# Layer 1's down step with seven block products for some pairs, and ELU from Relu and Exp

## Chip, cores and metric

The kernel runs on one core of a Trainium2 chip. The metric is the time of one execution in microseconds (us) of device time, and lower is better. The kernel before takes 1011.63 us, the median of three runs (1011.47 to 1011.79).

## The reference

There are 6016 tokens and 256 channels. An attention over channels comes first: q and k are divided by their column norms, `a = softmax(k^T q / tau)` is 256x256, and the tokens become `v @ a`. Two layers follow, each with 2048 hidden columns:

```python
h = x @ w_in                                   # [6016,256] @ [256,2048]
g = where(h > 0, h, exp(minimum(h, 0)) - 1)    # layer 1: ELU;  layer 2: g = h / (1 + exp(-h))
y = g @ w_out                                  # [6016,2048] @ [2048,256]
```

All is float32. TensorE (PE) works on `fp32r` operands. Each operand is split in two parts, hi (rounded) and lo (the rest), and a product is three matmuls: hi hi, hi lo and lo hi (`PARTS`).

## The kernel before

`a` is folded into layer 1's first weights (`a_w_in1 = a @ w_in1`, eight pieces), so that layer 1 starts at v itself. Layer 1 runs over 12 token tiles, ten of 512 tokens and the last two of 448 (`ONE`). Its hidden columns are 16 f blocks of 128. One tile and one f block make a unit.

For each unit, PE runs `up` (2 channel blocks times 3 parts, six matmuls of 512 columns, into one of four PSUM banks). ScalarE (ACT) writes Exp of the bank to `g_raw` (L728). VectorE (DVE) takes `min(e, 1) - 1` (L953) and then `max(h, 0) + that` (L957). ACT copies the result, rounded, to the hi part (`g_hi`, L700), and DVE subtracts for the lo part (`g_lo`, L911). Three units later PE runs `down`: for two output blocks c, three matmuls each, summed over all 16 f blocks in the tile's own bank (six matmuls of 512 columns). So a unit is 12 matmuls, and PE's order is up(f), down(f-3), up(f+1), down(f-2). ACT and DVE have loops of their own over the same units and do other work in fixed slots: the split of the finished tile's output (`y1_hi_of`, `y1_lo_of`), the transposition and split of the next tile of v (`v_transpose`, `vT_hi`, `vT_lo`), in tile 0 the split of seven more weight pieces (`weights_hi`, `weights_lo`, slots `SLOTS_WEIGHTS`), in tiles 1 to 4 two pairs each of the weight sums that layer 2 needs (`form_sums`, `form_hi`, `form_lo`). Every engine takes its instructions in order; semaphores join them.

Layer 2 (`TWO`, six double tiles) takes f blocks in pairs and already computes its down step with seven products of half-size blocks in place of eight (a Strassen-Winograd scheme): sums of g quarters (`pair_sums`) and of weight blocks (`w_out2_forms`) are multiplied, and sums of the seven results (`c_sums`) give the outputs. Its pairs go through a ring of four weight buffers that SyncE (SP) loads.

Of the kernel before, what the change touches and what calls it, by code (L numbers as in the profile page):

```python
# [63 lines left out]
M7, M5, M6, M4, M1, M2, M3 = range(N_PRODUCTS)  # L64

# [8 lines left out]
FIRST_H = (0, 1, 2, 3, 4, 0, 4, 5)  # L74
# [7 lines left out]
def build(nc, q, k, v, tau, w_in1, w_out1, w_in2, w_out2, out):  # L82
# [16 lines left out]
    assert N % P == 0 and C == 2 * P and F % WC == 0 and FB % N_H == 0  # L99

    ctx = ExitStack()
    with ctx:
# [16 lines left out]
        xb = [[place(f"x_parts{b}{a}", [P, 2, CB, T], F32R) for a in range(2)] for b in range(2)]  # L119
# [34 lines left out]
        assert at_wout1 + 2 * N_PRODUCTS * T * 4 <= at_x and at_g + 2 * N_PRODUCTS * T * 4 <= at_y1
        cursor[0] = at_x
        ring += [place(f"w_forms{r}", [P, N_PRODUCTS, 2, P], F32R) for r in range(1, N_RING)]
        assert cursor[0] <= at_g
        cursor[0] = at_g + 2 * N_PRODUCTS * T * 4
        mc = place("m_tile", [P, N_PRODUCTS + 2, T], F32)
        o_sb = place("out_tile", [P, 2, G, CB, BLK], F32)  # L160
# [4 lines left out]
        wraw = place("early_w_in1_parts", [P, 2, CB, F], F32R, at_win2_parts)  # L165

# [3 lines left out]
        cursor[0] = at_g  # L170
# [93 lines left out]
        class Phase:  # L264
# [21 lines left out]
        for t in range(NT):  # L286
            ONE.append(Phase(t // 2, t % 2, T_LAST if t >= NT - 2 else T, ONE[-1] if ONE else None))
# [3 lines left out]
        IN_LOOP_1, IN_LOOP_2 = range(6, NT - 4), range(1, NU - 1)  # L291
        assert len(IN_LOOP_1) % 2 == len(IN_LOOP_2) % 2 == 0

        def phases_one(eng, one):

            for ph in ONE[:IN_LOOP_1[0]]:
                one(ph)
            with eng.Fori(0, len(IN_LOOP_1) // 2) as i:
                half = i + IN_LOOP_1[0] // 2
                a = Phase(half, 0, before=Phase(half - 1, 1))  # L300
                one(a)
                one(Phase(half, 1, before=a))
            for ph in ONE[IN_LOOP_1[-1] + 1:]:
                one(ph)
# [22 lines left out]
        unit = lambda ph, f: ph.tile * FB + f  # L327

# [120 lines left out]
        def _(sp):  # L449
# [96 lines left out]
            weight_load(IN2 + 2)  # L546
            weight_load(IN2 + 3)
            v_load(2)
            form_load(0)
            for t in range(1, IN_LOOP_1[0]):  # L550
                spill(t - 1)
                if 2 * t - 1 < PAIRS:
                    form_load(2 * t - 1)
                    form_spill(2 * t - 2)
                v_load(t + 2)
                if 2 * t <= PAIRS:
                    if 2 * t < PAIRS:
# [69 lines left out]
        def _(act):  # L627
# [70 lines left out]
            def g_hi(ph, f):  # L698
                act.wait_ge(u_g, unit(ph, f) + 1)
                act.activation(gp[:, f % N_H, 0, 0:ph.n], g_sb[:, f % 2, 0:ph.n], ACT.Copy).then_inc(u_hi, 1)  # L700

            def y1_hi_of(ph):


                if ph.fixed == 0:
                    act.wait_ge(w_split, n_split(IN2 + N_PIECES - 1))
                else:
                    act.wait_ge(d_spill, 16 * ph.tile)
                for c in range(CB):
# [12 lines left out]
            def phase_one(ph):  # L722
                for f in range(FB):
                    act.wait_ge(u_up, unit(ph, f) + 1)

                    if not (ph.fixed == 0 and f < 2):
                        act.wait_ge(u_lo, unit(ph, f) - 1)
                    act.activation(g_sb[:, f % 2, 0:ph.n], h_ps[f % N_H][:, 0:ph.n], ACT.Exp).then_inc(u_act, 1)  # L728
                    if shifted(ph, f, 1):
                        g_hi(*shifted(ph, f, 1))  # L730
                    if f == SLOT_EVICT and ph.before:
                        y1_hi_of(ph.before)
                    if f == SLOT_V + 1 and ph.v_next:
                        vT_hi(*ph.v_next)
                    if weights_in_slot(ph, f) is not None:
                        weights_hi(act, weights_in_slot(ph, f))
                    if f and pair_in_slot(ph, f - 1) is not None:
                        form_hi(pair_in_slot(ph, f - 1))

            phases_one(act, phase_one)  # L740
# [36 lines left out]
            def tile(u):  # L777
                for k in range(PAIRS):
                    back = shifted(u, k, 1, PAIRS)
                    if u is TWO[0] and k == 0:  # L780
                        g_hi(ONE[-1], FB - 1)
# [10 lines left out]
                    if u is TWO[0] and k == 1:  # L792
                        y1_hi_of(ONE[-1])
# [524 lines left out]
```

## Time and profile before

| | us |
|---|---|
| median of three runs | 1011.63 |
| profiled execution | 1011.59 |
| its span, first to last instruction | 1009.8 |
| PE busy | 1004.0 (99%) |
| PE weight loads (PEld) busy | 894.7 (89%) |
| DVE busy | 781.7 (77%) |
| ACT busy | 577.2 (57%) |

Busy time is the union of an engine's instructions. A matmul's record is longer than the step to the next matmul, since matmuls overlap in the array. DVE and ACT instructions overlap a little too, so the step from start to start is shorter than the duration.

### The profile page before, as it was taken

The page shows a single profiled execution, that of the slowest core. Times are in us where ns is not written, and L with a number is a line of the kernel's source. Part 1 is how long each engine was busy: PE and PEld are TensorE (multiplying, and loading weights), DVE is VectorE, ACT ScalarE, POOL GpSimd, SP SyncE. Part 2 cuts the span into 40 slices and gives each one's busy share as a digit, 9 for nine tenths or more (in the row PEclk, how much of TensorE's full clock was granted, in tenths as well). Part 3 has the DMA queues.
Part 4 walks back from the last instruction along what each step waited for, and adds up shares of the span by engine and source line. Part 5 has one row for each costly group of instructions (what it writes and reads, how often), then busy time and mean ns, then how long its engine had stood idle before and what let it go on. Part 6 is the DMA issues. An engine that isn't in the chain of part 4 may idle for free.

```text
span 1009.8 us, 13274 instructions
## 1 busy us (share of the span) xinstructions
PE 1004.0 (99%) x4750; PEld 894.7 (89%) x4750; DVE 781.7 (77%) x1106; ACT 577.2 (57%) x916; POOL 10.2 (1%) x11
## 2 busy tenths in 40 slices
PE   9999999999999999999999999999999999999998
PEld 8888888888888888889999888888888888888997
DVE  7789878778777776777775866877887886886886
ACT  6766555555544444454445656656666665666664
POOL 0300000000000000000000000000000000000000
PEclk9999999999999999999999999999999999999999
DMA  9912313233111121114103325236237236334333
GB/s 350 373 17 73 110 53 104 102 102 110 74 27 43 21 63 42 19 53 175 42 37 146 110 74 192 89 92 238 73 95 229 93 93 203 109 93 130 110 97 91
DMA packets 115062, 109.77 MB, mean 109 GB/s; under 512 B 89024, under 2 KB 97216, under 8 KB 112448
## 3 DMA queue, kind: packets, MB, share of 16 engines
q1 hardware_dynamic: 114400, 108.58, 33.2%
q8 instruction: 32, 0.52, 0.2%
q10 hardware_dynamic: 608, 0.49, 0.2%
q14 instruction: 22, 0.18, 0.1%
HBM read 83.23 MB, written 25.82 MB: 108 GB/s over the span
## 4 chain that ended last, share of the span: by engine, by line
PE 97%; DMA 1%; ACT 1%; DVE 0%; issue 0%; SPq 0%; DVEq 0%
PE bank L1110 73%; PE bank L1257 21%; PE bank L1120 2%; DMA early_w_in<-w_in 1%; DMA early_qk<-k 0%; PE bank L1289 0%; ACT g_pair L751 0%; ACT g_pair_parts L758 0%; PE bank L1297 0%; DVE m_tile L1089 0%; ACT g_pair_parts L765 0%; SPq L461 0%; ACT early_w_in_parts L368 0%; PE bank L1153 0%; DVE out_tile L1100 0%
## 5 line engine op out<-in xcount | busy, mean ns | idle before, releaser
L1110 PE MATMUL bank<-g_parts,w_out_parts 128*128 128x512 f32 (+1 forms) x1152 | 274.9, 375 | 0.0
L1110 PE MATMUL bank<-x_parts,w_in_parts 128*128 128x512 f32 (+1 forms) x1152 | 274.5, 375 | 0.2 <-ACT g_pair L751 0.2
L1110 PE MATMUL bank<-xT_parts,a_w_in 128*128 128x512 f32 (+1 forms) x1152 | 274.5, 375 | 0.0
L728 ACT ACTIVATE g_raw<-bank 128x512 f32<-128x512 f32 (+1 forms) x192 | 112.8, 588 | 234.5 <-PE bank L1110 222.8
L1110 PEld LDWEIGHTS bank<-x_parts,w_in_parts 128*128 128x128 f32 x1152 | 215.9, 189 | 28.5 <-ACT g_pair L751 1.0
L1110 PEld LDWEIGHTS bank<-xT_parts,a_w_in 128*128 128x128 f32 x1152 | 217.9, 189 | 25.8
L1110 PEld LDWEIGHTS bank<-g_parts,w_out_parts 128*128 128x128 f32 x1152 | 218.0, 189 | 25.5
L1257 PE MATMUL bank<-g_pair_parts,w_forms 128*128 128x512 f32 (+1 forms) x987 | 239.3, 375 | 0.0
L1257 PEld LDWEIGHTS bank<-g_pair_parts,w_forms 128*128 128x128 f32 x987 | 186.8, 189 | 21.9
L751 ACT ACTIVATE g_pair<-bank 128x512 f32<-128x512 f32 (+1 forms) x192 | 112.9, 588 | 133.8 <-PE bank L1110 126.6
L953 DVE TENSOR_SCALAR g_raw<-g_raw 128x512 f32<-128x512 f32 (+1 forms) x192 | 80.2, 418 | 93.1 <-ACT g_raw L728 92.2
L911 DVE TENSOR_TENSOR g_parts<-g_raw,g_parts 128x512 fp32r<-128x512 f32 (+1 forms) x192 | 130.4, 679 | 12.8 <-ACT g_parts L700 0.8
L997 DVE TENSOR_TENSOR g_pair_parts<-g_forms,g_pair_parts 128x1024 fp32r<-128x1024 f32 (+1 forms) x96 | 115.1, 1200 | 21.6 <-ACT g_pair_parts L758 21.6
L957 DVE SCALAR_TENSOR_TENSOR g_raw<-bank,g_raw 128x512 f32<-128x512 f32 (+1 forms) x192 | 129.2, 673 | 0.0
L758 ACT ACTIVATE g_pair_parts<-g_forms 128x1024 fp32r<-128x1024 f32 (+1 forms) x96 | 99.2, 1035 | 34.4 <-PE bank L1257 33.3
L700 ACT ACTIVATE g_parts<-g_raw 128x512 fp32r<-128x512 f32 (+1 forms) x192 | 117.8, 614 | 1.2 <-DVE g_raw L957 1.2
L984 DVE TENSOR_TENSOR g_forms<-g_pair 128x1024 f32<-128x1024 f32 (+1 forms) x48 | 57.7, 1202 | 66.3 <-ACT g_pair L751 66.2
L1003 DVE TENSOR_TENSOR g_pair_parts<-g_pair,g_pair_parts 128x1536 fp32r<-128x1536 f32 (+1 forms) x48 | 82.5, 1718 | 2.0 <-ACT g_pair_parts L765 2.0
L765 ACT ACTIVATE g_pair_parts<-g_pair 128x1024 fp32r<-128x1024 f32 (+1 forms) x96 | 78.8, 822 | 0.6 <-PE bank L1257 0.6
L1120 PE MATMUL bank<-early_qk 128*128 128x256 f32 x188 | 41.3, 380 | 0.2 <-DMA early_qk<-k 0.2
L1120 PEld LDWEIGHTS bank<-early_qk 128*128 128x128 f32 x188 | 35.6, 191 | 5.1 <-DMA early_qk<-q 0.4
L821 DVE TENSOR_TENSOR early_square_sums<-early_square_sums,early_squares 128x1024 f32<-128x1024 f32 (+1 forms) x24 | 28.9, 1203 | 8.3 <-ACT early_squares L645 6.1
(84 smaller groups left out, 358.2 us busy)
## 6 DMA issues: line engine op xcount, KB each, us to landing
w_forms<-w_forms SPq DMA_DIRECT2D x48, 896.0 KB, 4.7
y_parts<-y1T_parts SPq DMA_DIRECT2D x10, 1024.0 KB, 3.9
x_parts<-y_parts SPq DMA_DIRECT2D x10, 1024.0 KB, 8.5
w_forms<-w_out_forms SPq DMA_DIRECT2D x8, 896.0 KB, 4.8
early_qk<-q SPq DMA_DIRECT2D x23, 256.0 KB, 7.4
early_qk<-k SPq DMA_DIRECT2D x22, 256.0 KB, 7.8
out<-out_tile SPq DMA_DIRECT2D x40, 128.0 KB, 2.7
v_in<-v SPq DMA_DIRECT2D x36, 128.0 KB, 3.4
```

The source lines that it names most:

```text
L700: act.activation(gp[:, f % N_H, 0, 0:ph.n], g_sb[:, f % 2, 0:ph.n], ACT.Copy).then_inc(u_hi, 1)
L728: act.activation(g_sb[:, f % 2, 0:ph.n], h_ps[f % N_H][:, 0:ph.n], ACT.Exp).then_inc(u_act, 1)
L751: act.activation(g2[:, k % 2, i, 0:u.n], h_bank(u, k, i)[:, 0:u.n], ACT.Silu).then_inc(u_act, 1)
L758: act.activation(gp2[k % 2][:, 0, 3 + 2 * s:5 + 2 * s, 0:u.n], t_sb[:, 2 * s:2 * s + 2, 0:u.n], ACT.Copy).then_inc(t_hi, 1)
L911: dve.tensor_tensor(part(1), g_sb[:, f % 2, 0:ph.n], part(0).bitcast(F32), ALU.subtract).then_inc(u_lo, 1)
L953: dve.tensor_scalar(g, g, 1.0, 1.0, ALU.min, ALU.subtract).then_inc(u_em, 1)
L957: dve.scalar_tensor_tensor(g, h_ps[f % N_H][:, 0:ph.n], 0.0, g, ALU.max, ALU.add).then_inc(u_g, 1)
L997: dve.tensor_tensor(part(1), t_sb[:, 2 * s:2 * s + 2, 0:u.n], part(0).bitcast(F32), ALU.subtract).then_inc(t_lo, 1)
L1003: dve.tensor_tensor(part(1), g2[:, k % 2, 1:4, 0:u.n], part(0).bitcast(F32), ALU.subtract).then_inc(r_lo, 1)
L1110: mm = pe.matmul(dst, lhsT, rhs, start=first and n == 0, stop=last and n == len(todo) - 1)
L1120: mm = pe.matmul(s_ps[i][:, 0:C], qk[c % NQ][:, K, r, i * P:(i + 1) * P], qk[c % NQ][:, Q, r, :], start=c == 0 and r == 0, stop=c == NCH - ...
L1257: mm = pe.matmul(m_banks[m][:, 0:u.n], ring[k % N_RING][:, form, x, :], by_turns(gp2[k % 2][:, y, operand, 0:u.n]), start=k == 0 and part ...
```

## The change

Layer 1 now works in pairs of f blocks, eight slots to a tile, and PE's lag is two pairs. Tile 0 has no pair with seven products; tiles 1 to 8 have three (pairs 0, 2, 4), tiles 9 to 11 four (0, 2, 4, 6). The others are plain: 12 down matmuls of a full tile. A pair with seven products takes the tile's two token halves and the pair's two f blocks as quarters of g (256 columns each, 224 in the last two tiles). DVE makes four sums of quarters (`one_sums`), ACT rounds three quarters and the four sums, DVE makes their lo parts, and PE runs 21 matmuls of 256 columns. The seven results lie in halves of banks 4 to 7; ACT copies one bank (`one_copy`), DVE makes the output halves (`y_sums`) and adds the plain pairs' sums (`y_rows`). The four weight sums for four pairs are made once, in tile 0 (`one_forms_*`).

ELU becomes: ACT writes `relu(-h)` (`relu`), then `exp(-that)` in place (`exp`), and DVE takes `max(e - 1, h)` for the whole pair in one instruction of 1024 elements (`one_g`).

Layer 2's weight sums move from two pairs a tile in tiles 1 to 4 to one a tile in tiles 1 to 8. The loops of layer 1 are written out. Several buffers move, and with them the first loads of layer 2: the tokens of its second tile wait for the last output of layer 1, its first two ring loads for layer 1's last pair but one, the next two for its last pair.

```diff
-SLOTS_WEIGHTS = (1, 3, 5, 8, 10, 12, 14)
+SLOTS_WEIGHTS = (1, 2, 3, 4, 5, 6, 7)
+SLOT_ONE_FORMS_SUM, SLOT_ONE_FORMS_HI, SLOT_ONE_FORMS_LO = 5, 6, 7
-FORM_PHASES = (1, 2, 3, 4)
+FORM_PHASES = (1, 2, 3, 4, 5, 6, 7, 8)
+SLOT_FORM_SUM, SLOT_FORM_HI, SLOT_FORM_LO = 0, 2, 6
+SLOT_V_TURN, SLOT_V_HI, SLOT_V_LO = 4, 5, 6
+SLOT_ROWS, SLOT_Y1_HI, SLOT_Y1_LO = 2, 3, 4
+COPY_LAG, SUM_LAG = 3, 4
+ONE_PRODUCTS = (M1, M5, M7, M6, M2, M3, M4)
+WINO_FEW, WINO_MORE = (0, 2, 4), (0, 2, 4, 6)
-FIRST_H = (0, 1, 2, 3, 4, 0, 4, 5)
+FIRST_H = (0, 1, 2, 3, 0, 1, 2, 3)
...
+            def relu(ph, k, i):
+                f = 2 * k + i
+                act.wait_ge(u_up, unit(ph, f) + 1)
+                if one_pair(ph, k) >= 2:
+                    act.wait_ge(u_lo, 2 * one_pair(ph, k) - 2)
+                act.activation(raw_units(ph, k)[:, i, :], h_ps[f % 4][:, 0:ph.n], ACT.Relu, scale=-1.0).then_inc(u_relu, 1)
+            def exp(ph, k, i):
+                act.wait_ge(u_relu, unit(ph, 2 * k + i) + 1)
+                e = raw_units(ph, k)[:, i, :]
+                act.activation(e, e, ACT.Exp, scale=-1.0).then_inc(u_act, 1)
+            def normal_hi(ph, k):
+                act.wait_ge(u_g, one_pair(ph, k) + 1)
+                pair_free(ph, k)
+                act.activation(gpn[k % 2][:, 0, :, 0:ph.n], raw_units(ph, k), ACT.Copy).then_inc(u_hi, 2)
...
+            def slot_one(ph, k):                       # ScalarE
+                if ph.tile == 1 and k == SLOT_ROWS:
+                    y1_hi_of(ONE[0])
+                back = shifted(ph, k, 1, PAIRS)
+                is_wino = back is not None and back[1] in back[0].wino
+                if is_wino:
+                    one_plain_hi(*back)
+                relu(ph, k, 0)
+                if is_wino:
+                    one_sums_hi(*back)
+                elif back:
+                    normal_hi(*back)
+                exp(ph, k, 0)
+                relu(ph, k, 1)
+                exp(ph, k, 1)
...
+                if ph.tile > 1 and k == SLOT_Y1_HI:
+                    y1_hi_of(ph.before)
+                if k == SLOT_V_HI and ph.v_next:
+                    vT_hi(*ph.v_next)
+                if weights_in_slot(ph, k) is not None:
+                    weights_hi(act, weights_in_slot(ph, k))
+                if ph.tile == 0 and k == SLOT_ONE_FORMS_HI:
+                    one_forms_hi()
...
+            def one_g(ph, k):
+                dve.wait_ge(u_act, unit(ph, 2 * k + 1) + 1)
+                g = raw_units(ph, k)
+                dve.scalar_tensor_tensor(g, g, -1.0, two_banks[k % 2][:, :, 0:ph.n], ALU.add, ALU.max).then_inc(u_g, 1)
...
+            def slot_one(ph, k):                       # VectorE
+                back = shifted(ph, k, 1, PAIRS)
+                if ph.tile == 1 and k == SLOT_ROWS:
+                    y1_lo_of(ONE[0])
+                if back:
+                    one_g(*back)
+                for tile in (ph, ph.before):
+                    if tile and tile.wino and k + PAIRS * (tile is not ph) == tile.wino[-1] + SUM_LAG:
+                        y_sums(tile)
+                if ph.tile > 1 and k == SLOT_ROWS:
+                    y_rows(ph.before)
+                if back:
+                    one_pair_parts(*back)
+                if ph.tile > 1 and k == SLOT_Y1_LO:
+                    y1_lo_of(ph.before)
+                if k == SLOT_V_TURN and ph.v_next:
+                    v_transpose(*ph.v_next[:2])
+                if k == SLOT_V_LO and ph.v_next:
+                    vT_lo(*ph.v_next)
+                if weights_in_slot(ph, k) is not None:
+                    weights_lo(dve, weights_in_slot(ph, k))
+                if ph.tile == 0 and k == SLOT_ONE_FORMS_SUM:
+                    one_forms_sums()
+                if ph.tile == 0 and k == SLOT_ONE_FORMS_LO:
+                    one_forms_lo()
+                if form_pair(ph) is not None and k == SLOT_FORM_SUM:
+                    form_sums(form_pair(ph))
+                if form_pair(ph) is not None and k == SLOT_FORM_LO:
+                    form_lo(form_pair(ph))
...
+                if f % 2 == 0 and one_pair(ph, f // 2) >= 2:        # TensorE, up()
+                    pe.wait_ge(u_g, one_pair(ph, f // 2) - 1)
...
+            for ph in ONE:
+                for k in range(PAIRS):
+                    up(ph, 2 * k)
+                    up(ph, 2 * k + 1)
+                    if shifted(ph, k, LAG_PAIRS, PAIRS):
+                        one_down(*shifted(ph, k, LAG_PAIRS, PAIRS))
```

`one_sums` is three DVE instructions of 512, 256 and 256 elements that wait for each other, `one_plain_lo` two (512, 256), `one_sums_lo` one of 1024; `one_plain_hi` and `one_sums_hi` are their ACT counterparts. `normal_lo` is one DVE instruction of 1024. `y_sums` is 256, 256 and 512 elements, one waiting for the other, `y_rows` twice 512. `one_forms_sums` is four instructions of 512, `one_forms_hi` and `one_forms_lo` two each of 1024.

## Rows read from the trace of the kernel before

**Rows 1.** The page's first part: busy us (share) x instructions of each engine.
```profile
PE 1004.0 (99%) x4750; PEld 894.7 (89%) x4750; DVE 781.7 (77%) x1106; ACT 577.2 (57%) x916; POOL 10.2 (1%) x11
```
**Rows 2.** The page's chain that ended last, by engine.
```profile
PE 97%; DMA 1%; ACT 1%; DVE 0%; issue 0%; SPq 0%; DVEq 0%
```
**Rows 3.** Busy time by stretch: us, PE, PEld, DVE, ACT, POOL, clock, DMA, GB/s.
```profile
58.50:100.00 41.50, 41.50 (x194) 36.40 (x193) 37.92 (x62) 27.01 (x43) 0.00 (x0) 1.00 0.18 45
341.40:382.90 41.50, 41.50 (x194) 36.36 (x194) 30.50 (x53) 19.94 (x37) 0.00 (x0) 1.00 0.14 39
```
**Rows 4.** PE's timeline in layer 1: start, us, what (512 and 448 columns).
```profile
352.45 1.46 PE L1110 MATMUL bank<-xT_parts,a_w_in 128*128 128x512 f32 x6
355.04 1.46 PE L1110 MATMUL bank<-xT_parts,a_w_in 128*128 128x512 f32 x6
...
537.58 1.30 PE L1110 MATMUL bank<-xT_parts,a_w_in 128*128 128x448 f32 x6
539.85 1.30 PE L1110 MATMUL bank<-xT_parts,a_w_in 128*128 128x448 f32 x6
```
**Rows 5.** The timeline of short matmuls and of weight loads in the early stage.
```profile
47.03 1.04 PE L1153 MATMUL bank<-ident,v_in 128*128 128x128 f32 x8
...
40.69 0.63 PEld L1131 LDWEIGHTS bank<-ones,early_square_sums 128*128 128x128 f32 x4
41.24 4.62 PEld L1120 LDWEIGHTS bank<-early_qk 128*128 128x128 f32 x22
```
**Rows 6.** Groups by shape: line engine op, shapes, count, busy us, mean ns.
```profile
L1110 PEld LDWEIGHTS bank<-g_parts,w_out_parts 128*128 128x128 f32 x1152 | 218.0, 189 | 25.5
L1120 PE MATMUL bank<-early_qk 128*128 128x256 f32 x188 | 41.3, 380 | 0.2 <-DMA early_qk<-k 0.2
L1153 PE MATMUL bank<-ident,v_in 128*128 128x128 f32 x8 | 1.0, 272 | 0.0
```
**Rows 7.** ACT's timeline in layer 1, tile 7 and tile 0.
```profile
351.36 0.60 ACT L728 ACTIVATE g_raw<-bank 128x512 f32<-128x512 f32 x1 [1.48 <-PE bank L1110]
351.85 0.62 ACT L700 ACTIVATE g_parts<-g_raw 128x512 fp32r<-128x512 f32 x1
352.37 1.07 ACT L711 ACTIVATE y1T_parts<-bank 128x512 fp32r<-128x512 f32 x2
...
62.34 1.04 ACT L368 ACTIVATE w_out_parts<-early_w_out 128x1024 fp32r<-128x1024 f32 x1
63.28 0.58 ACT L728 ACTIVATE g_raw<-bank 128x512 f32<-128x512 f32 x1
```
**Rows 8.** DVE's timeline in layer 1, tile 7, and in layer 2.
```profile
351.99 0.43 DVE L953 TENSOR_SCALAR g_raw<-g_raw 128x512 f32<-128x512 f32 x1 [0.78 <-ACT g_raw L728]
352.51 0.69 DVE L911 TENSOR_TENSOR g_parts<-g_raw,g_parts 128x512 fp32r<-128x512 f32 x1
353.12 0.68 DVE L957 SCALAR_TENSOR_TENSOR g_raw<-bank,g_raw 128x512 f32<-128x512 f32 x1
...
647.05 1.23 DVE L997 TENSOR_TENSOR g_pair_parts<-g_forms,g_pair_parts 128x1024 fp32r<-128x1024 f32 x1 [0.53 <-ACT g_pair_parts L758]
648.20 1.22 DVE L1026 TENSOR_TENSOR m_tile<-m_tile 128x1024 f32<-128x1024 f32 x1
```
**Rows 9.** Groups by shape on DVE and ACT, shorter ones, and a table load.
```profile
L943 DVE TENSOR_TENSOR w_out_forms<-form_stage,w_out_forms 128x256 fp32r<-128x256 f32 x8 | 3.4, 419 | 0.0
L929 DVE TENSOR_TENSOR w_out_form_sums<-form_stage 128x128 f32<-128x128 f32 x8 | 2.3, 284 | 0.0
L997 DVE TENSOR_TENSOR g_pair_parts<-g_forms,g_pair_parts 128x896 fp32r<-128x896 f32 x16 | 17.3, 1089 | 2.8 <-ACT g_pair_parts L758 2.8
L751 ACT ACT_TABLE_LOAD x1 | 1.3, 1283 | 0.0
```
**Rows 10.** Waits in tile 0 (58 to 101 us): total, times, longest.
```profile
ACT g_raw L728 <- DVE g_parts L911: 11.7, 9, 1.5
```
**Rows 11.** The page's DMA issues: count, KB each, us to landing.
```profile
w_forms<-w_forms SPq DMA_DIRECT2D x48, 896.0 KB, 4.7
```

More of the change, by code:

```diff
@@ L154, in build @@
[L154 to L158, printed above, removed]
+        assert cursor[0] <= at_forms1
+        ring = [place(f"w_forms{r}", [P, N_PRODUCTS, 2, P], F32R) for r in range(2)]
+        assert cursor[0] <= at_e
+        cursor[0] = at_e
+        ring += [place(f"w_forms{r}", [P, N_PRODUCTS, 2, P], F32R) for r in range(2, N_RING)]
@@ L290, in build @@
         LAST = TWO[-1]
[L291 to L304, printed above, removed]
+        IN_LOOP_2 = range(1, NU - 1)
+        assert len(IN_LOOP_2) % 2 == 0
         def tiles_two(eng, one):
@@ L702, in y1_hi_of, with one_copy @@
+            def one_copy(ph):
+                act.wait_ge(p1_down, one_pair(ph, ph.wino[-1]) + 1)
+                if ph.tile >= 2:
+                    act.wait_ge(y1_lo, CB * ph.tile)
+                act.activation(y_sum(ph, slice(Y_P1, Y_P5 + 1, Y_P5 - Y_P1)),
+                               bank[4][:, 0:ph.n].rearrange("p (s x) -> p s x", s=2), ACT.Copy).then_inc(m1_copy, 1)
             def y1_hi_of(ph):
-                if ph.fixed == 0:
+                if ph.tile == 0:
                     act.wait_ge(w_split, n_split(IN2 + N_PIECES - 1))
+                    act.wait_ge(p1_down, PAIRS)
@@ L714, in form_hi, with one_forms_hi @@
+            def one_forms_hi():
+                act.wait_ge(f1_sum, 4)
+                for i in range(2):
+                    act.activation(forms1[:, 2 * i:2 * i + 2, :, 0, :], form1_raw[:, 2 * i:2 * i + 2, :, 1, :],
+                                   ACT.Copy).then_inc(f1_hi, 1)
             def form_hi(k):
@@ L720, in form_hi @@
                 act.activation(forms[:, b, A11, 0, :], form_stage[:, 0, 0, :], ACT.Copy).then_inc(f_hi, 1)
[L722 to L738, printed above, removed]
@@ L973, in pair_sums @@
+            for ph in ONE:
+                for k in range(PAIRS):
+                    slot_one(ph, k)
             def pair_sums(u, k, step):
@@ L1049, in tile @@
                     if u is TWO[0] and k == 0:
-                        g_lo(ONE[-1], FB - 1)
+                        one_g(ONE[-1], PAIRS - 1)
+                        one_pair_parts(ONE[-1], PAIRS - 1)
+                    if u is TWO[0] and k == 1:
+                        y_sums(ONE[-1])
                     if back:
@@ L1071, in tile @@
                         plain_lo(*back)
-                    if first:
+                    if u is TWO[0] and k == 3:
                         y1_lo_of(ONE[-1])
```

397 lines of the change are left out of this document (268 added, 129 removed).

## The prediction, made before the changed kernel was run

> **What bounds the kernel now.** I read the page's engine shares first, then the chain that ended last, then busy time by stretch. PE is busy for 1004.0 of 1009.8 us [rows 1], and 97% of the chain is PE [rows 2]: the reader is to see that a change pays only through PE's matmuls, and costs only what makes PE wait. In layer 1 PE is busy in every microsecond of a tile [rows 3], at the full 2.4 GHz clock. Twelve matmuls of 512 columns take 355.04 - 352.45 = 2.59 us, 0.216 each; twelve of 448 take 2.27 us, 0.189 each [rows 4]. So a tile of 16 units is 41.4 us, one of the last two 36.3. In those 41.4 us DVE has 30.5 us of work and ACT 19.9; in tile 0 DVE has 37.9 [rows 3], and ACT waits nine times for DVE's lo parts there [rows 10]. The two are not idle helpers: I take them as the second bound.
>
> **PE's part.** A pair with seven products replaces 12 matmuls of 512 columns by 21 of 256. No row has an fp32r matmul of 256 columns, so I bound its step. From below: eight short PE transpositions, of 272 ns each [rows 6], step by (1.04 - 0.27) / 7 = 0.110 us [rows 5], each with its own weight load; the straight line through the 512 and 448 column steps (0.027 us per 64 columns) gives 0.109 at 256. From the weight loads: the four of L1131 belong to matmuls of one column, so nothing but the loads can space them. From the first of them (40.69) to the next group (41.24) are 0.55 us; the first waits out one fp32 matmul (0.216, 41.3 us over 188 is 0.220 [rows 6]), the other three are (0.55 - 0.216) / 3 = 0.111 us apart [rows 5]. From above: a load's own record, 0.189 us [rows 6]. I take 0.111, where the nearest rows meet. Then a pair is 21 x 0.111 = 2.33 instead of 2.59: 0.26 us gained, in 8 x 3 + 4 = 28 pairs 7.2 us. With 224 columns the load's 0.111 stays the floor: 2.33 against 2.27, 0.06 lost in each of 8 pairs. One plain matmul a tile is cut in two, under 0.01 us. PE alone would gain 7.2 - 0.5 = 6.7 us.
>
> One rule of the Trainium skill speaks against even this. "Perfetto Trace Analysis", section "Identifying the Most-Contended Engine", judges TensorE's headroom by the summed time of its LDWEIGHTS records. By it 21 x 0.189 = 3.97 us would be the cost of a pair, and the change a loss. The rows do not bear it out: four records of 0.19 fit in 0.63 us [rows 5], so records overlap and their sum is no occupancy. It is the third rival.
>
> **What ACT and DVE now have to do in a slot.** An instruction occupies its engine from start to start: ACT 0.49 us for 512 elements from a bank, 0.52 from SBUF, 0.94 for 1024; its result is there after 0.60, 0.62, 1.05 [rows 7]. DVE: 0.61 and 1.15, results after 0.69 and 1.22 [rows 8]; 256 elements give 0.42, 128 give 0.28 [rows 9]. A hand-over takes 0.03 (ACT ends at 351.96, DVE starts at 351.99 [rows 7, 8]). ELU by itself costs ACT one pass of 0.52 more a unit and saves DVE 0.34 + 0.61 - 0.575. Both engines have that time; what they don't have is the order. `one_g(k)` waits for `exp(k,1)`; ACT puts `normal_hi(k-1)` or `one_sums_hi(k-1)`, which wait for DVE, ahead of `exp(k,0)`, `relu(k,1)`, `exp(k,1)`. So from one `one_g` to the next there is a closed ring through both engines, and its length is the least time of a slot:
> - plain slot: one_g 1.22 + 0.03, normal_hi 0.94, exp 0.52, relu 0.60 + 0.03, exp 0.62 + 0.03 = 3.99 us;
> - slot with seven products: one_g 1.25, the three sums one after the other (0.69 + 0.42 + 0.42, with 0.03 each) 1.62, one_sums_hi 0.94, then 0.52 + 0.63 + 0.65 as above = 5.61 us.
>
> PE needs 5.18 for a plain slot and 2.59 + 2.33 = 4.92 for the other. The ring is longer in every slot with seven products.
>
> **Tiles 1 to 8.** Slot 0 is DVE's own: one_g 1.15, y_sums 1.51 (0.45 + 0.45 + 0.61), normal_lo 1.15, four form sums at 0.21 = 4.65. Slots 1, 3, 5: 5.61 each, 16.83. Slots 2 and 7: 3.99 each. In slots 4 and 6 DVE's queue is the length, since behind normal_lo (one_g 1.25, normal_hi 1.05 + 0.03, normal_lo 1.15, and 0.15 because y1_hi or vT_hi pushes normal_hi back) stand y1_lo 1.22 and v_transpose 1.15, or vT_lo 1.22 and form_lo 1.16: 6.0 each. The sum is 4.65 + 16.83 + 7.98 + 12.0 = 41.5 us. PE would need 41.43 - 3 x 0.26 = 40.65. So the tile is as long as before, +0.1: the matmuls' gain is spent waiting for `u_lo` and `u_g`. In 8 tiles +0.5 us. With hand-overs of 0.06 instead of 0.03 the eleven later tiles lose some 9 us more; with none they win 9.
>
> **Tile 0.** Here each of slots 1 to 7 has a weight piece, and it joins the ring: behind `exp(k,1)` ACT does weights_hi, DVE's weights_lo waits for that, and `one_g(k)` stands behind it. The ring is 1.25 + 0.94 + 0.52 + 0.63 + 0.52 + 1.05 + 0.03 + 1.15 = 6.09 us, while PE needs 5.18. Slot 5 adds vT_hi (1.04, ahead of weights_hi) and one_forms_sums (0.61 + 0.61 + 0.72 + 0.61 = 2.55): 9.68. Slot 7 adds one_forms_lo (2 x 1.15): 8.39. The seven are 4 x 6.09 + 9.68 + 6.09 + 8.39 = 48.5, for PE 36.3. There is no lead to eat into, because `up` of pair 2 already waits for `one_g(0)` (no down step lies between pairs 0, 1 and 2). So +12.2 us. Cover that is gone: before, PE's `up` didn't wait for `u_g` and the pieces lay seven in sixteen slots. In tile 1 PE's first product in banks 6 and 7 waits for y1_lo of tile 0, which follows its last down by two passes on each engine: +1.0.
>
> **Tiles 9 to 11.** Tile 9: four slots of 5.61, two of 4.0, one of 6.0, one of 4.85 (slot 6 without forms): 41.3, -0.1. Tiles 10 and 11: instructions of 896 instead of 1024 elements save 0.13 [rows 9], those of 448 0.07, so the slots are 5.1 (four), 3.6, 4.5 (y_sums and y_rows together), 5.3 and 4.3: 38.2 against 36.3, twice +1.9 = +3.8.
>
> **Layer 2's start and SP.** The last tile's plain hi, y_sums and y_rows (1.51 + 1.22 and 0.9 us more than before) now lie beside layer 2's first slots. Ring loads 0 and 1 start with the end of layer 1's last seven-product pair, about 7.4 us before layer 2's first down, and take 4.7 [rows 11]; the second double tile's tokens, now behind the last spill, have a whole double tile. I take +1 us, between 0 and +4. On SP `v_load(2)` now stands ahead of the last weight load, but both wait for tile 0's slots 4 and 5 and are used after 7. The form loads, one a tile, wait for nothing late.
>
> Relu has no row. If it shared no table with Exp, each switch would be 1.28 us [rows 9], hundreds of us in all. Copy stands between Exps in every unit without one. The Trainium skill, "ScalarE: Activation LUTs", section "Table sets: the hidden batching unit", has relu in every set; no run here shows it. I take nothing.
>
> **Sum.** 12.2 + 1.0 + 0.5 - 0.1 + 3.8 + 1.0 = +18.4 us. PE's own gain of 6.7 is inside these tile lengths. The profiled execution took 1011.59 (span 1009.8), the median is 1011.63: 1030.0.
>
> **The rivals.**
> - *Only tile 0 pays* (chance 0.15). Later tiles run at PE's pace, because the ring is 2% over it and a little more overlap than I read takes that away. -6.7 + 12.2 + 1.0 + 1.0 = +7.5: 1019. For it: the margin is 0.85 us a tile. Against it: every term is a mean with little spread.
> - *Faster* (0.11): the ring binds nowhere, tile 0's pieces hide as they do now (seven pieces, PE busy throughout [rows 3]), and PE gets its 6.7 less 0 to 1: 1005. It decides at slot 1 of tile 0: if one_g's step there is under 5.18. Against it: that ring is read off the order of instructions.
> - *Short matmuls are dear* (0.10). If loads of 0.189 space them, PE needs 41.43 + 3 x 1.38 = 45.6 in tiles 1 to 8 (+33), +5.5 in tile 9, +1.7 x 8 = 13.6 in the last two, with tile 0 and the rest 1077. Or only 224 columns are dear: run like plain fp32, in four passes (256 columns take two records of 0.216 each, [rows 6]), a step of 0.432 x 224 / 256 = 0.378, 21 of them 7.9 instead of 2.27, +41: 1071.
> - *Table switches* (0.02): over 1100.
>
> The forecast itself has 0.62, from 1019 to 1042 by the hand-overs and layer 2's start. **Range** 1010 to 1042: it takes in the first rival, and leaves out the faster case and the dear ones. No change means within 0.2%, 2 us, about what a measurement of this kernel can tell. Faster by more 0.12, within 0.03, slower by more 0.85.
>
> **What would show it.** Starts of one_g in tile 0 6.1 us apart, and PE idle there for some 12 us, with DVE as releaser; tile length 41.5 in tiles 2 to 8, with PE idle 0.8 us a tile; 21 short matmuls in 2.33 us; no more table loads than three; the last two tiles 38 each. The prediction is wrong if PE is busy throughout tile 0, or if short matmuls step by more than 0.12.

## The result and the profile after

The changed kernel takes 1069.97 us (median of four runs, 1068.86 to 1070.87) against 1011.71 for the kernel before on the same chip: ratio 1.0574 [1.0556, 1.0593], 58.3 us slower. The prediction was 1030.0, slower by 18.4, with a range up to 1042. The direction is right, the size isn't.

The page's first part and its chain, beside [rows 1] and [rows 2]:
```profile
PE 1023.8 (96%) x5085; PEld 904.8 (85%) x5085; DVE 831.3 (78%) x963; ACT 722.0 (68%) x1097; POOL 10.2 (1%) x11
...
PE 42%; DVE 23%; ACT 15%; issue 9%; DVEq 0%; ACTq 0%
```
PE no longer is the bound: the chain's share of PE fell from 97% to 42%, and DVE and ACT carry 38%. Busy time by stretch, with the columns of [rows 3]; the first stretch is tile 0 and tile 1, the second the rest of layer 1 but its last slots, the third layer 2's start:
```profile
58.00:160.00 102.00, 92.82 (x434) 78.14 (x434) 72.35 (x86) 70.46 (x111) 0.00 (x0) 0.97 0.17 46
160.00:580.00 420.00, 394.29 (x2104) 350.48 (x2103) 338.24 (x444) 310.28 (x510) 0.00 (x0) 0.98 0.19 57
580.00:640.00 60.00, 55.26 (x271) 48.39 (x270) 43.74 (x50) 38.47 (x57) 0.00 (x0) 0.97 0.22 85
```
PE idles 9.2, 25.7 and 4.7 us in these stretches. What PE waited for, total, times and longest:
```profile
PE banks L1314 <- DVE g_raw L1015: 23.2, 14, 4.2
PE banks L1452 <- DVE g_form_parts L1049: 5.6, 7, 1.1
PE banks L1452 <- DVE y_sums L1084: 3.9, 9, 0.6
PE banks L1314 <- ACT g_pair L850: 2.6, 3, 1.7
PE banks L1314 <- ACT g_raw L749: 2.1, 1, 2.1
```
In the first line `up` waits for `one_g` (L1015), from which the prediction counts its slots. These are, from start to start of `one_g`:

| tile | slots 0 to 7, us | sum | forecast |
|---|---|---|---|
| 0 | 6.17 6.14 6.14 6.15 9.71 6.15 8.41 4.53 (`one_g` of pairs 0 to 7) | 53.4 | 6.09, 9.68, 8.39 named |
| 3 | 4.73 5.65 4.07 5.65 **9.37** 5.62 6.02 4.05 | 45.2 | 4.65 5.61 3.99 5.61 **6.0** 5.61 6.0 3.99 = 41.5 |

Tiles 2 to 7 are alike within 0.3 us. From `one_g` of pair 0 to that of the next tile, tile 8 takes 44.5, tile 9 44.5, tile 10 41.3. Seven of tile 3's eight slots are within 0.1 us of the forecast. Slot 4 is not: 9.3 to 9.4 for 6.0, in tiles 2 to 9. In tile 10 it takes 7.5, in tile 11 6.0, both for a forecast of 5.3.

PE's timeline around such a slot (tile 5), beside [rows 4] and [rows 5]:
```profile
310.77 0.50 PE L1452 MATMUL banks<-g_form_parts,w_out_parts 128*128 128x256 f32 x3
...
313.11 2.76 PE L1314 MATMUL banks<-xT_parts,a_w_in 128*128 128x512 f32 x12
315.70 2.75 PE L1428 MATMUL banks<-g_parts,w_out_parts 128*128 128x512 f32 x12
320.35 2.86 PE L1314 MATMUL banks<-xT_parts,a_w_in 128*128 128x512 f32 x12 [1.90 <-DVE g_raw L1015]
```
The 21 short matmuls of a pair take 313.11 - 310.77 = 2.34 us, 0.111 each, as forecast. Then PE is idle for 1.90 us until `one_g` at 319.13 has ended. The two engines ahead of it, ACT and DVE, beside [rows 7] and [rows 8]:
```profile
309.60 2.78 ACT L791 ACTIVATE y1T_parts<-y_sums 128x512 fp32r<-128x512 f32 x2
312.29 0.58 ACT L744 ACTIVATE g_raw<-banks 128x512 f32<-128x512 f32 x1
312.77 1.05 ACT L759 ACTIVATE g_parts<-g_raw 128x1024 fp32r<-128x1024 f32 x1
```
```profile
309.73 1.22 DVE L1015 SCALAR_TENSOR_TENSOR g_raw<-g_raw,banks 128x1024 f32<-128x1024 f32 x1 [0.44 <-ACT g_raw L749]
313.92 1.23 DVE L1020 TENSOR_TENSOR g_parts<-g_raw,g_parts 128x1024 fp32r<-128x1024 f32 x1 [2.97 <-ACT g_parts L759]
315.06 2.98 DVE L1090 TENSOR_TENSOR y1T_parts<-y_sums,y1T_parts 128x512 fp32r<-128x512 f32 x2
317.97 1.22 DVE L939 STREAM_TRANSPOSE v_transposed<-v_in 128x1024 f32<-128x1024 f32 x1
319.13 1.17 DVE L1015 SCALAR_TENSOR_TENSOR g_raw<-g_raw,banks 128x1024 f32<-128x1024 f32 x1
```
`y1_hi` (L791) takes 2.78 us for two passes, where [rows 7] has 1.07; it holds back `normal_hi` (L759), so DVE is idle for 2.97. Then `y1_lo` (L1090) takes 2.98 for two. The operation, the number of elements and the step of the read (every fourth element, 16 bytes) are those of before. What differs is where they read: before, a PSUM bank; now `y_sums`, in SBUF. Tile 0 of the changed kernel has no `y_sums`; its output is still read from the banks, with the same step, by the same two lines, which take there what they took before:
```profile
121.89 1.07 ACT L791 ACTIVATE y1T_parts<-banks 128x512 fp32r<-128x512 f32 x2
122.51 1.29 DVE L1090 TENSOR_TENSOR y1T_parts<-banks,y1T_parts 128x512 fp32r<-128x512 f32 x2 [0.92 <-ACT y1T_parts L791]
```

### The profile page after: what moved, and what is told of

Same layout as the page of the kernel before. It is cut to its first block, busy times and chain, and to the rows that moved or that the text cites. A ratio compares the mean times of both kernels' runs of the same rounds, so it can differ in the third digit from the quotient of the medians.

```text
span 1069.1 us, 14152 instructions
## 1 busy us (share of the span) xinstructions
PE 1023.8 (96%) x5085; PEld 904.8 (85%) x5085; DVE 831.3 (78%) x963; ACT 722.0 (68%) x1097; POOL 10.2 (1%) x11
## 4 chain that ended last, share of the span: by engine, by line
PE 42%; DVE 23%; ACT 15%; issue 9%; DVEq 0%; ACTq 0%
PE banks L1314 22%; PE banks L1511 19%; ACT g_raw L749 6%; DVE g_raw L1015 5%; ACT g_raw L744 3%; DVE g_parts L1020 3%; ACT y1T_parts L791 2%; DVE g_raw_forms L1031 2%; ACT g_parts L759 2%; DVE y1T_parts L1090 2%; DVE g_form_parts L1043 2%; DVE g_raw_forms L1034 1%; DVE g_raw_forms L1036 1%; DVE v_transposed L939 1%; DVE g_form_parts L1044 1%
## 5 line engine op out<-in xcount | busy, mean ns | idle before, releaser
L1314 PE MATMUL banks<-xT_parts,a_w_in 128*128 128x512 f32 (+1 forms) x1152 | 271.3, 387 | 23.3 <-DVE g_raw L1015 23.2
L1314 PE MATMUL banks<-x_parts,w_in_parts 128*128 128x512 f32 (+1 forms) x1152 | 276.4, 376 | 4.7 <-ACT g_pair L850 2.6
L1314 PEld LDWEIGHTS banks<-xT_parts,a_w_in 128*128 128x128 f32 x1152 | 220.3, 195 | 56.9 <-DVE g_raw L1015 26.4
L1314 PEld LDWEIGHTS banks<-x_parts,w_in_parts 128*128 128x128 f32 x1152 | 215.9, 190 | 34.6 <-ACT g_pair L850 4.5
L1511 PE MATMUL banks<-g_pair_parts,w_forms 128*128 128x512 f32 (+1 forms) x987 | 239.3, 375 | 0.0
L1511 PEld LDWEIGHTS banks<-g_pair_parts,w_forms 128*128 128x128 f32 x987 | 186.5, 189 | 22.1
L850 ACT ACTIVATE g_pair<-banks 128x512 f32<-128x512 f32 (+1 forms) x192 | 112.9, 588 | 134.6 <-PE banks L1314 127.8
L1428 PE MATMUL banks<-g_parts,w_out_parts 128*128 128x512 f32 (+1 forms) x709 | 162.6, 376 | 0.0
L1428 PEld LDWEIGHTS banks<-g_parts,w_out_parts 128*128 128x128 f32 x709 | 133.7, 190 | 16.3
L1015 DVE SCALAR_TENSOR_TENSOR g_raw<-g_raw,banks 128x1024 f32<-128x1024 f32 (+1 forms) x96 | 114.5, 1193 | 25.0 <-ACT g_raw L749 25.0
L1020 DVE TENSOR_TENSOR g_parts<-g_raw,g_parts 128x1024 fp32r<-128x1024 f32 (+1 forms) x60 | 72.4, 1207 | 69.1 <-ACT g_parts L759 68.6
L749 ACT ACTIVATE g_raw<-g_raw 128x512 f32<-128x512 f32 (+1 forms) x192 | 118.1, 615 | 3.1
L759 ACT ACTIVATE g_parts<-g_raw 128x1024 fp32r<-128x1024 f32 (+1 forms) x60 | 62.6, 1043 | 56.0 <-issue 47.8
```

What stands on the lines that cost most here:

```text
L749: act.activation(e, e, ACT.Exp, scale=-1.0).then_inc(u_act, 1)
L759: act.activation(gpn[k % 2][:, 0, :, 0:ph.n], raw_units(ph, k), ACT.Copy).then_inc(u_hi, 2)
L850: act.activation(g2[:, k % 2, i, 0:u.n], h_bank(u, k, i)[:, 0:u.n], ACT.Silu).then_inc(u_act, 1)
L1015: dve.scalar_tensor_tensor(g, g, -1.0, two_banks[k % 2][:, :, 0:ph.n], ALU.add, ALU.max).then_inc(u_g, 1)
L1020: dve.tensor_tensor(part(1), raw_units(ph, k), part(0).bitcast(F32), ALU.subtract).then_inc(u_lo, 2)
L1314: mm = pe.matmul(dst, lhsT, rhs, start=first and n == 0, stop=last and n == len(todo) - 1)
```

## The experiments

**Is it the way `y_sums` is read?** e1 reads it in order and leaves out the turn of the tokens that the output needs. e2 keeps the turn: it reads `y_sums` in order and writes with a step of 512 bytes; its `y1_lo` also reads the hi part with that step.
```diff
-    act.activation(y1T[...].rearrange("p (m b) -> p m b", m=4), turned_back(y_raw(ph, c), 4), ACT.Copy)
+    # e1, tiles from 1 on; y1_lo alike
+    act.activation(y1T[...].rearrange("p (m b) -> p m b", m=4), y_raw(ph, c).rearrange("p (m b) -> p m b", m=4), ACT.Copy)
+    # e2
+    act.activation(y1T[...].rearrange("p (m b) -> p b m", m=4), y_raw(ph, c).rearrange("p (b m) -> p b m", m=4), ACT.Copy)
```


> The changed kernel, with the two passes that split a layer 1 output tile (y1_hi, y1_lo) reading it in order instead of every fourth element; the tokens' order within tiles 1 to 11 is left out, all else is the same. Theory (the passes themselves are dear, because they now read SBUF with a step of 16 bytes: 1.41 and 1.48 us instead of 0.59 and 0.68 from a bank): the passes fall to about 0.62 and 0.69, slot 4 (one_g to one_g) from 9.4 to 6.0 us, tiles 2 to 8 from 45.2 to 41.6, in all 31 us less: 1039. Rival (slot 4 is long because ACT and DVE stand in the wrong order, and because PE's clock falls): passes shorter, but slot 4 stays above 8 us, and the time above 1060.

> The changed kernel, whole, with the same two passes reading the tile in order and writing y1T with a step of 512 bytes between neighbours (the lo pass also reads the hi part with that step). If only reading with a step of 16 bytes is dear, the passes are 0.62 and 0.69 us and the time is that of the kernel without the turn, 1039. If any step in SBUF costs this much, the time stays at 1070.

Measured: e1 1035.8 us, ratio to before 1.024 [1.0223, 1.0257]; e2 1052.51, 1.0402 [1.0385, 1.042]. The groups of the passes (count, busy us, mean ns), in after, e1 and e2:
```profile
L791 ACT ACTIVATE y1T_parts<-y_sums 128x512 fp32r<-128x512 f32 (+1 forms) x22 | 29.0, 1368 | 0.0
L1090 DVE TENSOR_TENSOR y1T_parts<-y_sums,y1T_parts 128x512 fp32r<-128x512 f32 (+1 forms) x22 | 30.4, 1426 | 0.0
```
```profile
L793 ACT ACTIVATE y1T_parts<-y_sums 128x512 fp32r<-128x512 f32 (+1 forms) x22 | 12.3, 604 | 0.0
L1094 DVE TENSOR_TENSOR y1T_parts<-y_sums,y1T_parts 128x512 fp32r<-128x512 f32 (+1 forms) x22 | 13.9, 673 | 0.0
```
```profile
L796 ACT ACTIVATE y1T_parts<-y_sums 128x512 fp32r<-128x512 f32 (+1 forms) x22 | 21.9, 1098 | 0.0
L1099 DVE TENSOR_TENSOR y1T_parts<-y_sums,y1T_parts 128x512 fp32r<-128x512 f32 (+1 forms) x22 | 22.2, 1053 | 0.0
```
With the turn gone, slot 4 is 6.05 us and tile 3 41.85: 34 us of the 58 are the strided read. e2 lies between both expectations: ACT's pass, whose write alone has a step, takes 1.10 us, so a step on the writing side costs too, though less (slot 4 7.65).

**Is the step dear by itself?** e4 is the kernel before with eight DVE subtractions and eight ACT copies of 512 elements added behind its end, one after the other, reads with steps of 4, 8, 16, 32, 64 and 512 bytes and writes with 16 and 512.
```diff
+    dve.tensor_tensor(t_out(way), g_in(way), t_two(way), ALU.subtract)    # way: the step
+    act.activation(t_out(way), g_in(way), ACT.Copy)
```


> The kernel before, and behind its end on DVE eight subtractions and on ACT eight copies of 512 elements, one after the other: reading with steps of 4, 8, 16, 32, 64 and 512 bytes between neighbours, then writing with steps of 16 and 512. Its total time means nothing. Theory (a step of 16 bytes in SBUF reads is dear): the first two near 0.69 (DVE) and 0.62 (ACT), 16 bytes near 1.45 and 1.4. Open: the steps above 16 bytes, and the writes. Rival (the passes are slow in the changed kernel because other engines use the same memory at the time): all eight near 0.69 and 0.62 here.

Steps of 4, 8 and 16 bytes on DVE, then on ACT:
```profile
1006.59 0.68 DVE L1127 TENSOR_TENSOR g_forms<-g_pair 128x512 f32<-128x512 f32 x1
1007.30 0.69 DVE L1129 TENSOR_TENSOR g_forms<-g_pair 128x512 f32<-128x512 f32 x1
1008.03 1.06 DVE L1131 TENSOR_TENSOR g_forms<-g_pair 128x512 f32<-128x512 f32 x1
```
```profile
1014.52 0.63 ACT L820 ACTIVATE g_forms<-g_pair 128x512 f32<-128x512 f32 x1 [8.47 <-DVE g_forms L1141]
1015.18 0.66 ACT L822 ACTIVATE g_forms<-g_pair 128x512 f32<-128x512 f32 x1
1015.87 1.11 ACT L824 ACTIVATE g_forms<-g_pair 128x512 f32<-128x512 f32 x1
```
Every larger step, read or written, took 1.01 to 1.12 us. So a step of 16 bytes costs 0.38 on DVE and 0.48 on ACT, and a larger one about as much, in one execution with PE idle. That explains e2's passes, and only half (DVE) or some 60% (ACT) of what after's passes take more than e1's. In after itself the passes are shorter where PE's matmuls have 448 columns. Tile 9's lie in tile 10 (below); tile 10's, of 448 elements, lie in tile 11 and take 1.02 and 0.98 us each, while those of tile 11, also of 448 elements, lie in layer 2 beside matmuls of 512 columns and take 1.35 and 1.38.
```profile
534.58 2.19 ACT L791 ACTIVATE y1T_parts<-y_sums 128x512 fp32r<-128x512 f32 x2
539.15 2.11 DVE L1090 TENSOR_TENSOR y1T_parts<-y_sums,y1T_parts 128x512 fp32r<-128x512 f32 x2
```

**Who slows them further?** e8 puts PE beside them: four streams of matmuls behind the end of the kernel before. The kernel's matmuls read their moving operand interleaved, alternately from its first and its second half.
```diff
+    for n, turned, count in ((512, True, 60), (448, True, 68), (512, False, 60), (256, True, 116)):
+        x = gp2[0][:, 0, j % N_PRODUCTS, 0:n]
+        pe.matmul(bank[0][:, 0:n], ring[0][...], by_turns(x) if turned else x, ...)
```


> Edit: the kernel before, whole, and behind its last output four streams of fp32r matmuls on PE: 60 of 512 columns in the interleaved order of the kernel (its two runs 1024 bytes apart), 68 of 448 so (896 bytes apart), 60 of 512 in plain order, 116 of 256 interleaved. Beside each stream ACT makes four copies of 512 elements, then DVE four subtractions: twice with a 16-byte read step, once with a 512-byte step, once in order. Alone (PE idle) these took 1.11, 1.11, 1.08, 0.63 on ACT and 1.06, 1.06, 1.03, 0.68 on DVE; in the changed kernel the 16-byte passes took 1.41 and 1.48 beside matmuls of 512 columns and 1.10 and 1.06 where the last two tiles' matmuls of 448 ran. Theory A (the interleaved stream of 512 columns slows a read of 16-byte step, and the distance of its two runs matters): 1.4 and 1.5 in the first stream, 1.1 in the others. Theory B (any PE stream does it): 1.4 and 1.5 in all four. Theory C (it isn't PE's reads, but the other engine or the DMA queues of the running kernel): 1.1 in all four.

The first read of 16-byte step in each stream, on ACT and on DVE:
```profile
1008.71 1.59 ACT L826 ACTIVATE g_forms<-g_pair 128x512 f32<-128x512 f32 x1 [2.07 <-PE bank L1331]
...
1021.53 1.15 ACT L826 ACTIVATE g_forms<-g_pair 128x512 f32<-128x512 f32 x1 [7.81 <-PE bank L1331]
...
1034.60 1.11 ACT L826 ACTIVATE g_forms<-g_pair 128x512 f32<-128x512 f32 x1 [8.93 <-PE bank L1331]
...
1047.63 1.37 ACT L826 ACTIVATE g_forms<-g_pair 128x512 f32<-128x512 f32 x1 [8.93 <-PE bank L1331]
```
```profile
1013.75 1.53 DVE L1123 TENSOR_TENSOR g_forms<-g_pair 128x512 f32<-128x512 f32 x1 [6.48 <-ACT g_forms L826]
1025.70 1.10 DVE L1123 TENSOR_TENSOR g_forms<-g_pair 128x512 f32<-128x512 f32 x1 [7.02 <-ACT g_forms L826]
1038.74 1.07 DVE L1123 TENSOR_TENSOR g_forms<-g_pair 128x512 f32<-128x512 f32 x1 [8.97 <-ACT g_forms L826]
1052.27 1.34 DVE L1123 TENSOR_TENSOR g_forms<-g_pair 128x512 f32<-128x512 f32 x1 [9.51 <-ACT g_forms L826]
```
The second read of each stream agrees with the first within 0.02 us. Theory A holds for the 512 interleaved columns (halves 1024 bytes apart): 1.59 and 1.53. Neither 448 interleaved (896 bytes apart) nor 512 in plain order does it. It is not the whole rule: 256 interleaved columns (512 bytes apart) cost half as much, 1.37 and 1.34, which I had not expected. The reads with a 512-byte step in the same streams kept their 1.1 us. In these streams the distance of the halves goes with the number of columns, so which of the two matters isn't separated, and the reason stays open.

**Tile 0.** e3 moves each weight piece's lo part behind the next `one_g`.
```diff
+                if back and weights_in_slot(*back) is not None:    # DVE's slot_one, right behind one_g(*back)
+                    weights_lo(dve, weights_in_slot(*back))
...
-                if weights_in_slot(ph, k) is not None:
-                    weights_lo(dve, weights_in_slot(ph, k))
```


> The changed kernel, with each weights_lo on DVE one slot later, right behind the next one_g. Theory (in tile 0 the weight piece stands in the ring one_g, normal_hi, exp, relu, exp, weights_hi, weights_lo, one_g): the ring falls from 6.14 to about 4.0 us, tile 0 from 53.4 to some 42 us, PE's idle time of 4.2 us in slot 5 shrinks: 13 us less, 1057. Rival (DVE's and ACT's amount of work in tile 0 sets its length, not their order): no change, 1068 to 1071.

Measured: 1056.51 us, ratio 1.0438 [1.042, 1.0455]; tile 0 is 40.1 instead of 53.4. DVE's queue there in after, then in e3:
```profile
62.97 1.22 DVE L1015 SCALAR_TENSOR_TENSOR g_raw<-g_raw,banks 128x1024 f32<-128x1024 f32 x1 [2.41 <-ACT g_raw L749]
...
67.99 1.23 DVE L414 TENSOR_TENSOR w_out_parts<-early_w_out,w_out_parts 128x1024 fp32r<-128x1024 f32 x1 [1.32 <-ACT w_out_parts L408]
69.14 1.21 DVE L1015 SCALAR_TENSOR_TENSOR g_raw<-g_raw,banks 128x1024 f32<-128x1024 f32 x1
```
```profile
62.60 1.22 DVE L1015 SCALAR_TENSOR_TENSOR g_raw<-g_raw,banks 128x1024 f32<-128x1024 f32 x1 [2.42 <-ACT g_raw L749]
...
66.68 1.22 DVE L1015 SCALAR_TENSOR_TENSOR g_raw<-g_raw,banks 128x1024 f32<-128x1024 f32 x1 [0.37 <-ACT g_raw L749]
67.81 1.22 DVE L414 TENSOR_TENSOR w_out_parts<-early_w_out,w_out_parts 128x1024 fp32r<-128x1024 f32 x1
```
L414 no longer waits, and `one_g` no longer stands behind it.

**What is left, and which part of the change it is.** e5 repairs both costs: the turn is made where banks are read (`one_copy`, `y_sums`, `y_rows`), and the weight pieces' lo parts come later, as in e3. Besides, `one_sums_hi` leaves the ring. e6 has both repairs, ACT's order as in after and fewer seven-product pairs; e7 has none of these pairs, with the weight pieces later: ELU and the order by pairs alone.
```diff
 # e5, e6: y_rows; one_copy and y_sums alike. e5 also has ACT's order relu, exp, plain_hi, relu, exp, sums_hi
 # e5, e6, e7: also weights_lo as in e3
-    dve.tensor_tensor(y_raw(ph, c), y_banks[c][:, 0:ph.n], y_raw(ph, c), ALU.add)
+    raw = y_raw(ph, c).rearrange("p (a m b) -> p a m b", a=2, m=4)
+    dve.tensor_tensor(raw, y_banks[c][:, 0:ph.n].rearrange("p (a b m) -> p a m b", a=2, m=4), raw, ALU.add)
 # e6; e7: both ()
-WINO_FEW, WINO_MORE = (0, 2, 4), (0, 2, 4, 6)
+WINO_FEW, WINO_MORE = (0, 4), (0, 4, 6)
```


> Edit: the changed kernel with three repairs: the turn by four is made where the PSUM banks are read (one_copy, y_sums, y_rows), so y1_hi and y1_lo read runs of 64 or more elements; the weight pieces' lo parts one slot later, behind one_g; and in ACT's queue relu and exp of a pair's first unit stand ahead of plain_hi, sums_hi last. Theory (three separate costs: the strided passes 34 us, tile 0's ring 13.4, and what is left is the ring one_g, sums, sums_hi, exp of a seven-product slot): the first two give 1035.8 - 13.4 = 1022.4; with sums_hi out of the ring a seven-product slot falls from 5.65 to some 5.2, 3 or 4 such slots a tile, so 1018, between 1016 and 1020, and y1_hi and y1_lo take 0.62 and 0.69 us. Rival (the slot is the length of DVE's own queue, the order on ACT doesn't matter): 1022, slots of 5.6. Second rival (reading banks in the turned order costs as much as reading SBUF so): 1035 or more, one_copy and y_rows over 1 us.

> Edit: the changed kernel with the turn made at the banks and the weight pieces later, ACT's order left as changed, and two seven-product pairs a tile (0 and 4) in place of three, three (0, 4, 6) in place of four. Theory (a seven-product slot is longer on the ring than on PE, so each pair costs more than its matmuls give back): tiles 1 to 8 lose one slot of 5.65 each and the plain slots' 4.0 no longer pay for them; the tile goes back to PE's 41.4 - 2 x 0.26 = 40.9: 1022.4 less some 6 = 1016, between 1014 and 1019. Rival (seven-product pairs gain 0.26 us each and something else is left): eleven pairs fewer, so 1022.4 + 2.9 = 1025.

> Edit: the changed kernel without any pair of seven products (no forms of w_out1, no y_sums or y_rows, y1 read from the banks again, two alternating pairs of banks), with the weight pieces later: ELU in its new form and the order by pairs alone. Theory (ELU's extra ACT pass and the pair order cost nothing once tile 0's ring is gone): PE is the bound in every tile, 1011.7 as before plus 0 to 2 at layer 2's start: 1012, between 1011 and 1014. Rival (the pair order costs by itself, one_g being late for the up step in plain slots too): 1017 or more, PE idle in tiles 2 to 8 with one_g as releaser.

Measured: e5 1018.27, ratio 1.0059 [1.0043, 1.0076]; e6 1013.62, 1.0018 [1.0008, 1.0028]; e7 1012.57, 1.0007 [0.9998, 1.0017]. e5 and e7 lie in their ranges, e6 0.4 us below its own (1014 to 1019), on the side away from its rival, with tiles of 40.96 for 40.9. e7 can't be told from before: the extra ACT pass of ELU and the order by pairs cost nothing that can be measured here, 0.17% at most. In e5 the passes take 0.60 and 0.67 again, and a bank read in turned order is no dearer (`y_rows` 671 ns in after and in e5). But e5's 1018 came about in another way than its theory had it, and is luck to that extent: the seven-product slots of tile 3 take 5.50, 6.49 and 5.42 us and not 5.2 (in e1 5.65, 5.66 and 5.62), the two plain ones 3.63 and 3.60 (4.07 and 4.06), in sum 0.5 us less a tile. No run changes ACT's order alone. What remains there is the wait for the seven-product parts:
```profile
PE banks L1465 <- DVE g_form_parts L1054: 4.8, 12, 0.8
```
A tile with three seven-product pairs takes 41.3 us in e5 (41.85 in e1, which has ACT's order as in after), with two 40.96 in e6, with none 41.44 in e7. Busy time of such a tile in e6 and in e7, with the columns of [rows 3]:
```profile
225.73:266.68 40.95, 40.95 (x213) 36.47 (x212) 32.40 (x45) 30.80 (x52) 0.00 (x0) 1.00 0.24 68
```
```profile
182.97:224.41 41.44, 41.44 (x194) 36.29 (x193) 24.87 (x29) 28.69 (x47) 0.00 (x0) 1.00 0.23 67
```
PE is busy throughout in both. The last two tiles together take 71.3 from first to last `one_g` with three such pairs each (e6) and 68.6 with none (e7). So the pairs pay when there are two a tile and none at the end. That is e9:
```diff
-WINO_FEW, WINO_MORE = (0, 2, 4), (0, 2, 4, 6)
+WINO_FEW, WINO_MORE = (0, 4), (0, 4)
-                self.wino = () if tile == 0 else ...
+                self.wino = () if tile == 0 or n != T else ...    # on e6; the last two tiles' y1 from banks[4:6] and [6:8]
```


> Edit: the changed kernel with the turn made at the banks, the weight pieces later, seven-product pairs 0 and 4 in tiles 1 to 9 and none in the last two tiles, whose y1 is read from two alternating pairs of banks. Theory (a tile with two such pairs is 40.96 against 41.44 without any, and the last two tiles lose 2.6 with three): 1012.6 of the kernel without seven products less 9 x 0.48 = 1008.3, between 1007 and 1010, faster than before by 0.2 to 0.4%. Rival (the gain of a tile is given back at its ends: the banks of tile 9 come free late for tile 10, or layer 2's start): 1011 to 1013, PE idle at tile 10's first down step.

Measured: 1009.03 us, ratio 0.9972 [0.9962, 0.9982]: faster than both kernels, by 2.6 us than before. Its first part of the page, and 270 us of layer 1:
```profile
PE 1000.3 (99%) x4921; PEld 895.5 (89%) x4921; DVE 766.8 (76%) x863; ACT 689.5 (68%) x1059; POOL 10.2 (1%) x11
```
```profile
160.00:430.00 270.00, 270.00 (x1390) 240.42 (x1389) 213.78 (x283) 202.44 (x342) 0.00 (x0) 1.00 0.25 71
```
PE is busy throughout, at the full clock, and most of what 18 pairs can give, 18 x (2.59 - 2.34) = 4.5 us, arrives: 1004.0 - 1000.3 = 3.7 us less PE time, of which 2.6 show in the kernel's time.

## Why the prediction was wrong, step by step

- **PE's part** was right: 0.111 a step, also for 224 columns (537.29 to 539.62 for 21). The rival of dear short matmuls falls. The Trainium skill, "Perfetto Trace Analysis", section "Identifying the Most-Contended Engine", judges TensorE's headroom by the summed time of its load records. By that rule 21 loads, 195 ns each in this group, would need 4.1 us; the trace does not bear it out.
- **Tile 0** was right: 6.15 for 6.09, 9.71 for 9.68, 8.41 for 8.39, the seven slots 48.9 for 48.5. PE idles 8.1 us in it, not "some 12" (the other 1.1 of the first stretch lie in tile 1): behind its longest wait it ran at half clock (below) and so filled some 3 us in which it would have waited (an estimate: fifteen matmuls take 6.4 us there, from 98.55 on, for 3.2). e3 gives 13.5 back by the move that the argument names.
- **Slot 4 of tiles 2 to 8** is the step that failed: "y1_lo 1.22", and "0.15 because y1_hi or vT_hi pushes normal_hi back". `y1_lo` took 2.91 from start to start, +1.69; `normal_lo` waited 2.97 for 1.26 (0.03 + 1.05 + 0.03 + 0.15), +1.71; together the 3.4 by which the slot is longer. Of the 39.9 us by which the forecast was short (58.3 for 18.4), e1 gives 34.2 back by changing this read alone. The slot was rightly seen as DVE's queue behind `normal_hi`. The error was to take the passes' durations from rows of a bank [rows 7, 8] when the change moves their source to SBUF. No row of before showed such a strided read from SBUF, so, like the short matmuls, it needed bounds on both sides.
- **Tiles 9 to 11** carry the same passes: tile 9 44.5 for 41.3; tile 10 41.3 for 38.2, which e1 brings to 38.9.
- **Layer 2's start**: forecast +1.0. From the start of the last `one_g` to the end are 473.9 us, for 467.0 from the last `max(h, 0)` pass (L957) of before: +6.9; in e1 it is +2.7. `y1_hi` of the last tile stands ahead of layer 2's silu there, and PE waits for silu (L850, 2.6 us in the waits above, 0.2 in e1). So 4.2 of the 6.9 are the same strided read again, outside the +4 that I allowed.
- **The rest** holds: with the read repaired, e1 stands at 1035.8 for my 1030.0. Most of what is missing is 0.35 us in each of tiles 2 to 5 and 7 (41.85 for 41.5) and 0.6 in tile 6, 0.7 in tile 10, and 1.7 at layer 2's start.
- Of the **rivals**, tile 0 alone falls (with the read repaired, tiles 2 to 7 still take 41.85 in e1, where PE needs 40.65), and faster falls for the change as it is, though e9 shows that its mechanism exists. Table switches: there are none in layer 1.

## What to carry to other kernels

When a change moves an operand from PSUM to SBUF, price each pass anew, by its access step: the same ACT copy or DVE subtraction went from 0.6 to 1.1 us with a step of 16 bytes, and to 1.5 beside a certain PE stream. Put a reordering where a bank is read: there it cost nothing. And when two engines hand each other work in a ring near PE's own pace, count how many dear slots a tile can carry: here a tile took 41.44 us with none of eight, 40.96 with two, and 41.3 to 41.85 with three, by ACT's order.

## What the runs showed of the hardware that I had not expected

- A read of SBUF with a 16-byte step, 1.11 us on ACT and 1.06 on DVE with PE idle (e4), took 1.59 and 1.53 while PE ran matmuls of 512 columns that read two runs 1024 bytes apart alternately (e8).
- PE's clock fell after some idle stretches. Busy time by stretch in after, behind an idle stretch of 4.20 us and around one of 1.90:
```profile
98.50:104.00 5.50, 5.45 (x13) 4.37 (x14) 4.14 (x5) 5.39 (x7) 0.00 (x0) 0.50 0.16 46
...
320.00:325.00 5.00, 3.51 (x17) 2.84 (x18) 4.27 (x8) 4.42 (x8) 0.00 (x0) 1.00 0.93 201
```
In the first the granted clock is at its lower level, 1.2 GHz, and twelve matmuls take 5.49 us for 2.75. The second keeps 2.4 GHz, though another idle of 1.88 us, before 229.97, was followed by 0.66 on average (230 to 235 us). Of the eight tiles 2 to 9, each with such an idle stretch in slot 4 (1.75 to 2.12 us), four show a fall behind it; why these, stays open. In tiles 2 to 7 it cost nothing that can be seen: the tile with the 0.66 took 45.16 us, the one at full clock 45.20, because DVE and ACT set their length and not PE. In tile 10 it seems to have cost something: a fall from 528.0 to 531.4 lies in slot 3, which took 5.57 us, for 5.12 in e1 and e3, where the clock stayed up.
